# Seven products per pair in another order: an attention, MoE and MLP kernel on one core

## The reference

```python
attn_out = _attn_ref(q, k, v, mem_k, mem_v)       # 4 x 8 heads x 768 tokens x 64, chunks of 32
x = attn_out.transpose(0, 2, 1, 3).reshape(B * S, H * D)          # 3072 tokens x 512

h = x @ w_in                                      # _moe_ref, 512 -> 1024
e = np.exp(h - np.max(h, axis=-1, keepdims=True))
solu = h * (e / (np.sum(e, axis=-1, keepdims=True) + 1e-09))
ln = (solu - mu) / np.sqrt(var + 1e-06) * g_ln
x = ln @ w_out                                    # 1024 -> 512

h = x @ w_in                                      # _moe2_ref, 512 -> 2048
return np.maximum(0.01 * h, h) @ w_out            # 2048 -> 512
```

## Time and profile before

| | |
|---|---|
| median of the runs | 910.66 us |
| profiled execution, its own time | 911.71 us |
| its span, first to last instruction | 909.9 us |
| TensorE busy | 856.9 us, 94% |
| DVE, ACT busy | 553.4 us, 425.5 us |

### The profile page before, as it was taken

The page is one execution under the profiler, slowest core; times in us unless marked ns, Lnnn a source line. Parts: engine busy times, 40 slices in busy tenths (PEclk is TensorE's granted clock), DMA queues, the critical chain, the costliest instruction groups (busy, mean ns, idle before and its releaser), DMA issues.

```text
span 909.9 us, 13666 instructions
## 1 busy us (share of the span) xinstructions
PE 856.9 (94%) x5300; PEld 721.0 (79%) x5300; DVE 553.4 (61%) x990; ACT 425.5 (47%) x713; POOL 45.4 (5%) x84
## 2 busy tenths in 40 slices
PE   7999999999999897989988999899998999999998
PEld 6778888888888786778776788677776888888886
DVE  5686565656565743554465433455568969769875
ACT  4464444343434323353555544655563455445543
POOL 1111111101010110000000000000000000000000
PEclk9899999999999998999999999999999999999999
DMA  7752323233353513132757446843492273074001
GB/s 298 279 185 68 137 98 132 110 125 117 112 225 102 212 48 105 47 116 95 251 198 250 143 163 220 302 147 140 158 371 104 67 254 122 24 277 163 24 1 70
DMA packets 47921, 137.80 MB, mean 151 GB/s; under 512 B 4976, under 2 KB 9200, under 8 KB 43760
## 3 DMA queue, kind: packets, MB, share of 16 engines
q1 hardware_dynamic: 47856, 136.93, 42.0%
HBM read 92.87 MB, written 44.04 MB: 150 GB/s over the span
## 4 chain that ended last, share of the span: by engine, by line
PE 79%; DVE 7%; ACT 7%; issue 5%; DMA 2%; POOL 0%; SPq 0%; ACTq 0%; POOLq 0%; DVEq 0%
PE hid_ps L604 27%; PE x_ps L604 18%; PE ln_ps L604 9%; PE scores_ps L604 8%; PE attn_ps L604 5%; PE probs_ps L604 4%; PE scores_ps L570 2%; PE attn_ps L596 2%; PE ln_ps L634 1%; ACT g_out L745 1%; PE probs_ps L582 1%; ACT x_op_P_hi L745 1%; ACT lnT_hi L745 1%; DVE lnT_lo L1005 1%; DVE g_out L1127 1%
## 5 line engine op out<-in xcount | busy, mean ns | idle before, releaser
L745 ACT ACTIVATE ring_hi<-g_blk 128x512 fp32r<-128x512 f32 x168 | 106.0, 632 | 114.2 <-PE x_ps L604 45.8
L1005 DVE TENSOR_TENSOR ring_lo<-g_blk,ring_hi 128x512 fp32r<-128x512 f32 x168 | 115.5, 690 | 39.8 <-ACT ring_hi L745 35.7
L604 PE MATMUL x_ps<-lnT_hi,w_out_hi 128*128 128x384 f32 x256 | 88.9, 347 | 6.2 <-DVE lnT_lo L1005 5.0
L604 PE MATMUL x_ps<-lnT_hi,w_out_lo 128*128 128x384 f32 x256 | 86.4, 338 | 0.0
L604 PE MATMUL x_ps<-lnT_lo,w_out_hi 128*128 128x384 f32 x256 | 86.3, 337 | 0.0
L604 PE MATMUL hid_ps<-w_in_hi,xT_hi 128*128 128x512 f32 x192 | 79.3, 413 | 2.3 <-DVE u L1051 2.3
L871 ACT ACTIVATE g_out<-g_out 128x512 f32<-128x512 f32 x72 | 45.5, 632 | 75.0 <-DVE g_out L1127 28.1
L604 PE MATMUL hid_ps<-w_in_lo,xT_hi 128*128 128x512 f32 x192 | 77.2, 402 | 0.0
L604 PE MATMUL hid_ps<-w_in_hi,xT_lo 128*128 128x512 f32 x192 | 77.2, 402 | 0.0
L776 ACT ACTIVATE e<-hid_ps,neg_max 128x1024 f32<-128x1024 f32 x24 | 26.8, 1115 | 89.3 <-DVE neg_max L1045 89.2
L604 PE MATMUL hid_ps<-x_op_P_hi,w_hi 128*128 128x512 f32 x144 | 57.6, 400 | 10.6 <-ACT g_out L745 10.6
(11 more groups left out here) (150 smaller groups left out, 1918.9 us busy)
## 6 DMA issues: line engine op xcount, KB each, us to landing
attn_buf<-attn_in SPq DMA_DIRECT2D x32, 1152.0 KB, 6.8
g_scratch<-g_out SPq DMA_DIRECT2D x96, 256.0 KB, 2.7
g_blk<-g_scratch SPq DMA_DIRECT2D x48, 512.0 KB, 7.2
w_raw<-w_in SPq DMA_DIRECT2D x16, 512.0 KB, 4.0
x_scratch<-x_stage SPq DMA_DIRECT2D x8, 768.0 KB, 4.7
t_raw<-x_scratch SPq DMA_DIRECT2D x24, 256.0 KB, 5.4
t_scratch<-t_raw SPq DMA_DIRECT2D x24, 256.0 KB, 2.5
op_raw<-t_scratch SPq DMA_DIRECT2D x12, 512.0 KB, 5.5
```

The lines of the kernel that those rows point to most:

```text
L604: mm = pe.matmul(psum, weights[i], data[j], start=first and n == 0, stop=last and n == 2, skip_group_check=goes_on)
L745: return act.activation(dst, src, ACT.Copy)
L1005: return ve.tensor_tensor(dst, x, hi.bitcast(f32), ALU.subtract)
```

## The change

The order of TensorE in up, of ACT, of DVE and of SP, and of TensorE in the first span of down.

```diff
 def up_sequence():
     s = [(0, p) for p in ("P1", "P2", "P6", "P5", "P7")]
     for i in range(1, UPS):
-        s += [(i, "P1"), (i - 1, "P4"), (i, "P2"), (i - 1, "P3"), (i, "P6"), (i, "P5"), (i, "P7")]
+        s += [(i, "P1"), (i, "P2"), (i - 1, "P4"), (i, "P6"), (i, "P5"), (i - 1, "P3"), (i, "P7")]
     return s + [(UPS - 1, "P4"), (UPS - 1, "P3")]
+def op_slots(b):
+    return 4 if b else 3
+def down_steps(b):
+    def slices(p, first=0, last=PAIRS2):
+        return [(b, p, j) for j in range(first, last)]
+    if b == 0:
+        return (slices("P1") + slices("P2") + slices("P3", 0, 4) + slices("P6") + slices("P3", 4) + slices("P7") +
+                slices("P5") + slices("P4"))
+    return [step for p in ("P1", "P2", "P6", "P3", "P7", "P5", "P4") for step in slices(p)]
...
# schedule(), blocks 1 to 6
+        if t in (5, 6):
+            add(("t_sums", 0, t - 5))
         add(("scores", a + 2), ("shift", a + 2), ("expo", a + 2), ("rowsum", a + 2), ("probs", a + 2))
...
         elif t == 5:
-            add(("t_sums", 0, 0), ("t_sums", 0, 1), ("store_t", 0, 0), ("store_t", 0, 1), ("load_w2", 0))
+            add(("store_t", 0, 0))
+        elif t == 6:
+            add(("store_t", 0, 1))
...
# schedule(), block 7
-    add(("load_op", 0, 0), ("load_op", 0, 1), ("load_op", 0, 2))
+    add(("load_w2", 0), ("load_op", 0, 0), ("load_op", 0, 1), ("load_op", 0, 2))
+    add(("hidden_k", n, 0), ("hidden_k", n, 1))
     add(("ln_t", n - 1), ("split_ln", n - 1))
-    add(("hidden", n), ("neg_max", n), ("expo1", n))
-    add(("x2", t - 1, 0), ("stage_x2", t - 1, 0), ("solu", n), ("square", n), ("operand", 0, 0), ("w2_sum", 0),
+    add(("hidden_k", n, 2), ("hidden_k", n, 3), ("neg_max", n), ("expo1", n))
+    add(("x2", t - 1, 0), ("solu", n), ("square", n), ("stage_x2", t - 1, 0), ("w2_sum", 0), ("operand", 0, 0),
         ("load_op", 0, 3), ("stats", n), ("norm", n))
...
-    add(("x2", t - 1, 2), ("stage_x2", t - 1, 2), ("operand", 0, 2), ("load_op", 0, 5), ("load_w2", 1),
-        ("solu", n + 2), ("square", n + 2), ("operand", 0, 3), ("load_op", 0, 6), ("stats", n + 2), ("norm", n + 2))
+    add(("x2", t - 1, 2), ("solu", n + 2), ("square", n + 2), ("stage_x2", t - 1, 2), ("operand", 0, 2), ("load_op", 0, 5),
+        ("load_w2", 1), ("stats", n + 2), ("norm", n + 2), ("operand", 0, 3), ("load_op", 0, 6))
...
# PSUM of P3 in the first span of down
+        def p3_bank(b):
+            return down_z if b else down_x[1]
...
# TensorE, down
                     elif p == "P1" and b == 1:
-                        pe.wait_ge(s_c21, UPS)
+                        pe.wait_ge(s_d12, 2)
...
                     elif p == "P3":
-                        pe.wait_ge(s_d11, 2 * (b + 1))
+                        if b == 0:
+                            pe.wait_ge(s_c21, UPS)
+                        else:
+                            pe.wait_ge(s_d11, 2 * (b + 1))
...
# ACT, up
                 if i >= 2:
+                    leak22(i - 1)
                     keep1(i)
                 if border:
                     operand(b + 1, 0)
-                whole21(i - 1)
                 if i < PAIRS2 - 1:
                     w2_hi(i + 1)
-                if j == 0:
-                    operand(b, 5)
                 leak11(i)
                 if border:
                     operand(b + 1, 1)
-                leak12(i - 1)
+                whole21(i - 1)
                 if j == 0:
-                    operand(b, 6)
-                if i > UPS - PAIRS2:
-                    w2_hi(i - PAIRS2 - 1)
+                    operand(b, 5)
                 keep2(i)
                 if border:
                     operand(b + 1, 2)
                     operand(b + 1, 3)
                 if i == UPS - 1:
-                    ring_hi(0, 0, 0)
+                    ring_hi(0, "P1", 0)
+                leak12(i - 1)
+                if j == 0:
+                    operand(b, 6)
                 keep3(i)
-                leak22(i)
                 if border:
                     operand(b + 1, 4)
-            ring_hi(0, 0, 1)
+                if i > UPS - PAIRS2:
+                    w2_hi(i - PAIRS2 - 1)
+            leak22(UPS - 1)
+            ring_hi(0, "P1", 1)
+            ring_hi(0, "P1", 2)
+            w2_hi(2 * PAIRS2 - 1)
             whole21(UPS - 1)
...
# DVE, up
                 add11(i)
                 if i < PAIRS2 - 1:
                     w2_lo(i + 1)
+                if i < PAIRS2 - 2:
+                    w2_sum(i + 2)
+                if i >= UPS - PAIRS2 + 2:
+                    w2_lo(i - PAIRS2 - 2)
+                if i > UPS - PAIRS2:
+                    w2_sum(i - PAIRS2 - 1)
...
                 add12(i - 1)
...
-                if i > UPS - PAIRS2:
-                    w2_lo(i - PAIRS2 - 1)
...
                 add22(i)
-                if i < PAIRS2 - 2:
-                    w2_sum(i + 2)
-                elif i >= UPS - PAIRS2:
-                    w2_sum(i - PAIRS2)
...
# DVE, first span of down
+                if b == 0:
+                    if p == "P2":
                         t3(b, j)
+                    elif p == "P3" and j < 4:
+                        t2(b, 2 * j)
+                        t2(b, 2 * j + 1)
+                    elif p == "P3":
+                        t4(b, 2 * j - 8)
+                        t4(b, 2 * j - 7)
```

More of the change, by code:

```diff
@@ L314, in build @@
         s_t_out = [sem(f"s_t_out{k}") for k in range(2)]
-        s_op_in = [sem(f"s_op_in{i}") for i in range(3)]
+        s_op_in = [sem(f"s_op_in{i}") for i in range(4)]
         s_g_out = [{q: sem(f"s_g_out{s}_{q}") for q in (11, 12, 21, 22)} for s in range(2)]
@@ L735, in _ @@
                 up(i, p)
-            for b in range(SPANS):
-                for o in range(len(DOWN)):
-                    for j in range(PAIRS2):
-                        down(b, o, j)
+            for b, p, j in DOWN_STEPS:
+                down(b, p, j)
         @block.scalar
@@ L1190, in _ @@
                 border = j == PAIRS2 - 1 and b + 1 < SPANS
-                if border:
-                    operand(b + 1, 0)
                 add11(i)
@@ new lines, in _ @@
+            for b, p, j in DOWN_STEPS:
+                if DOWN_AT[b, p, j] >= RING:
+                    ring_low(b, p, j)
+                if b == 0:
+                    if p == "P2":
+                        t3(b, j)
+                    elif p == "P3" and j < 4:
[4 more added lines that the diff above has]
+                        t4(b, 2 * j - 7)
+                elif p == "P1":
+                    t3(b, j)
+                elif p == "P2":
+                    t2(b, j)
+                elif p == "P6":
+                    t4(b, j)
+                if p == "P7":
@@ L1257, in _ @@
                     t1(b, j)
-                for j in range(PAIRS2):
-                    ring_low(b, 5, j)
-                for j in range(PAIRS2):
-                    ring_low(b, 6, j)
+                if p == "P6" and j == 3:
+                    c11(b, 0)
+                    c11(b, 1)
+                if p == "P4":
                     if j in (1, 2):
```

233 lines of the change are left out of this document (105 added, 128 removed).

## The result

The changed kernel takes 874.36 us (median of 4 runs, 872.0 to 875.03), the kernel before 910.58 us in the same job (910.02 to 913.04). The ratio is 0.9593 [0.9567, 0.9619]: 4.1% faster. The prediction was 873 us, range 867 to 884. The profiled execution took 875.02 us, its span is 873.2 us, 36.7 us shorter than before.

A forecast was written before the change was run, and what follows sets the result against it. TensorE was taken to bound every stage from block 5 on, so only its idle time, restarts and low clock could give time. Terms 5.1 + 6.0 + 25.5 + 1.3 = 37.9 us off 911.71 gave a median of 873 us, range 867 to 884.

The forecast's parts named there:

- The step: Up: keep2 was held up by what stood before it; the new order gives it 1.9 us in hand before P7.
- the wrong remedy: Borders of up: with four slots operands 0 to 3 lie ready, and 5.3 us hide operand 4's load.
- the loss of 1.5 us forecast: Up: about 1.5 us of the 27.0 us lost would remain, so 25.5 us saved.
- Block 6: Block 6, with t_sums of span 0 moved, falls to block 5's 46.2 us: 5.1 us saved.
- Block 7: Block 7: shorter waits, one new wait and clock changes save 6.0 us, the least sure term; 3 or 9 possible.
- Only 0.5 us of it are new: Block 7: x2 group 3 waits some 3.5 us for stage_x2, but DVE's chain leaves only 0.5 us new.
- the waits of 5.26 and 3.00 us: Block 7: half a hidden tile fills 2.7 us of the first wait; the second goes, 3.3 us.
- Entrance of down: From up into down: new waits of 0.9, 1.3 and 1.0 us for ring_low plus restarts lose 3.7 us.
- the first rival: Entrance of down: the low clock comes in as TensorE idles, costing 1.7 us, for 874.5 us; chance 0.13.
- This term: First span of down: the loss falls from 5.8 to 0.8 us, 5.0 saved, net of the entrance 1.3 us.
- the prediction's sign for being wrong there: First span of down: the prediction is wrong if this span loses more than in the kernel before.
- The fourth: Up: the waits move to P6 in every pair because ACT is behind at keep1; 912 us or more, chance 0.03.

The follow-up runs named there:

- The first experiment: The kernel before, with only ACT's order in up edited: keep2 ahead of the previous pair's leak12 and of w2_hi; 897.75 us, ratio 0.9865.
- the experiment: The changed kernel with both t_sums of span 0 back at the end of block 5; 880.12 us, ratio 0.9676.
- The second experiment: The changed kernel with leak12 of the pair before back ahead of keep2 on ACT, the new order of products kept; 956.69 us, ratio 1.0514.

## Why the prediction was right, and where it was not

**Up.** The step held: `keep2` had been held up by what stood in front of it, and P7 waits for it no more, but for pair 2. Timeline of the changed kernel, `keep2` of a late pair and the P7 behind it: it ends at 608.71, 1.92 us ahead, for the 1.9 us of the prediction.

```profile
608.11 0.60 ACT L781 ACTIVATE g_out<-hid_ps 128x512 f32<-128x512 f32 x1 [0.30 <-PE hid_ps L640]
...
610.63 0.39 PE L640 MATMUL hid_ps<-x_op_P_hi,w_hi 128*128 128x512 f32 x1
```

The first experiment shows the cause apart from everything else. At the borders the prediction named the wrong remedy: it put the late loads down to the slots. The fourth slot is worth about 1 us, and preparing the operands a pair earlier, which it did not name, some 3.7 us. That the borders cost nothing, with 2.4 us kept for the range, was right: the changed kernel has no wait there. Of the loss of 1.5 us forecast (its own terms, 0.4 twice and 0.96, add up to 1.8) there are 2.4: the wait of 0.48 us in pair 2 was not on the list. Pairs 9 and 17 lose 0.3 us each, as forecast within 0.1. Behind the wait of pair 2 the chain of waits of the changed kernel has a store that took long to land:

```profile
421.50 6.75 DMA g_scratch<-g_out
```

**Block 6.** 5.1 us, and the experiment gives 5.1.

**Block 7.** The sum was right (6.6 for 6.0) by luck, since three of its steps were not. "Only 0.5 us of it are new": the whole 3.19 us are new; before, group 3 of `x2` followed without a wait. What paid for it was twofold. The clock gave 2.5 us, where 0.5 were forecast: TensorE was busy for 11.7 us at 0.50 in this block before and is for 6.7 now, and half of that is lost time. And there was a wait that the prediction had not seen, 1.98 us ahead of the third hidden tile. Timeline of the kernel before, DVE and the wait of TensorE behind it:

```profile
365.88 1.22 DVE L1005 TENSOR_TENSOR x_op_P_lo<-op_raw,x_op_P_hi 128x1024 fp32r<-128x1024 f32 x1 [2.87 <-ACT x_op_P_hi L745]
...
370.39 0.81 DVE L1069 TENSOR_SCALAR u<-u,neg_mean,gain 128x1024 f32<-128x1024 f32 x1 [0.93 <-POOL gain L1286]
...
374.89 0.50 PE L604 MATMUL hid_ps<-w_in_hi,xT_hi 128*128 128x512 f32 x1 [1.98 <-DVE u L1051]
```

An operand and the sums of a weight stood ahead of `norm`, and `neg_max` of the next tile behind it. In the changed kernel the sums of the weight stand ahead of the operand, and that wait is 0.16 us. The prediction took from this block the waits of 5.26 and 3.00 us alone.

**Entrance of down.** It lost 3.7 us, as forecast, in waits of 0.56, 1.23 and 0.91 us for 0.9, 1.3 and 1.0. The places and the causes were right. That the sum fits so well is luck: the forecast's three waits and three restarts of 0.31 us add up to 4.1, not 3.7, and the measured waits are shorter. The clock stayed at 1.00, so the first rival did not come in. The rule of the Trainium skill ("TensorE: Matmul & The Clock Gate", section "A second HAM failure mode: psum-queue depth-cycling"), that frequent short idles between groups of matmuls make the clock fall and rise again, is not borne out at this place. The second experiment agrees with it: there a wait of 1.93 us in every pair was followed by the lower clock in 18 of 23.

**First span of down.** This term failed: 0.8 us were to be lost, 2.0 are. The two costs (loads for `t3` 1.7 us late, DVE at 1.85 us over in four slices of P3) draw on the same 2.5 us of lead; together they are 1.05 us over it by the prediction's own figures. The load of `t3` 4 came late enough to use up the lead and 0.7 us more, and then the slices of P3 paid 1.3 us of DVE's rate; spreading `t2` takes those away. So the split of P3 saved 3.7 us and not 5.0. Entrance and first span together lose 5.9 us where the first span lost 5.8 before, so down gained nothing where 1.3 us were forecast, and the prediction's sign for being wrong there (more lost than before) was reached, if only by 0.1 us.

**The sum.** 37.9 us were forecast, and the two profiled executions are 36.7 apart (911.71 and 875.02). Down is 1.4 us under its forecast and up 1.0; block 7 is 0.6 over it, and 0.6 us came ahead of block 5, where nothing was changed.

**The rivals.** None took the place of the forecast. The fourth asked for a chain across engines that holds ACT up in every pair; the second experiment has one, and up takes 84 us longer with it.

## What to carry to other kernels

Where one engine takes work in a written order, look at what stands between an instruction and the value that it waits for, before touching the order of the engine that waits: here one line moved on ACT gave 15.5 of the 24.5 us in up. The new order of the waiting engine without its partner on ACT made up 84 us longer. A buffer's lead can be spent once: add up all that draws on it. And a store that frees a buffer should not stand behind loads that nobody wants yet.
